# Where a fused attention and two-layer FFN kernel does its second softmax and its first split

## Chip, cores and metric

The kernel runs on one core of one Trainium2 chip. The metric is the device time of one execution in microseconds (us), from start to end. Engines are called TensorE (PE), VectorE (DVE), ScalarE (ACT), GpSimd (POOL) and SyncE (SP).

## What is computed

A window attention with given weights (a softmax over 7 taps for each token and head, then a weighted sum of 7 neighbouring tokens), and two feed-forward layers on its result:

```python
w = weight_gen - np.max(weight_gen, axis=-1, keepdims=True)
w = np.exp(w)
w = w / (np.sum(w, axis=-1, keepdims=True) + 1e-09)
x_pad = np.concatenate([np.zeros((B, pad, D)), x], axis=1)   # pad = 6
...
out = np.einsum('bshk,bskhg->bshg', w, x_unf)                # B 2, S 4096, H 8, K 7, D 192
h = x @ w_in ; g = h * np.cos(h)      ; x = g @ w_out        # first layer, 192 -> 2048 -> 192
h = x @ w_in2; g = np.maximum(0.01*h, h); out = g @ w_out2   # second layer
```

## The kernel before

The 8192 tokens lie 64 to a partition; a chunk is 4 of these (J = 4), so there are C = 16 chunks of 512 tokens. Each FFN layer works through 8 units of 256 hidden columns. Float32 products are made of high and low parts: ScalarE rounds a copy to the high part, VectorE or GpSimd subtracts it from the value for the low part, and TensorE multiplies the parts in turn. TensorE fills a slot of PSUM (`fill_alone`, or `both_products`, which interleaves the fill of one unit with the sum of the unit three before it); ScalarE and VectorE turn the slot into `gate`, then `g_hi` and `g_lo`, and `both_products` or `sum_alone` adds it into `acc_a` and `acc_b`. Each engine has its own instruction list, written out by hand; order on an engine is the order of the code, and between engines semaphores decide.

What matters here is the start, before the steady loop. SyncE issues the loads in one list: the softmax weights of chunk 0 (`load_gen(0)`), the tokens of chunk 0 (`load_own(0)`), their halo, the 6 tokens before each partition's own (`load_halo`, four transfers), the columns of the first input matrix in three pieces (`load_columns`, `HI_PIECES`), with `load_gen(1)`, the softmax weights of chunks 1 and 2, behind the first piece. GpSimd issues the loads of the first output matrix (L638) after the last piece of columns has landed.

VectorE makes the softmax of chunk 0, then the attention of chunk 0 (`attention(0, dve)`): products with the taps (L318) and additions (L327). Its first item, `start`, needs only the chunk's own tokens (three products); the second, `rest_of_window`, waits for the halo. The semaphore `att` counts these, and TensorE, which must be kept busy for its clock, runs three dummy matmuls for each (`raise_clock`, L1381). When `att` is 11, TensorE transposes the tokens into a slot (`transpose_input`). ScalarE meanwhile rounds the columns (`column_highs_a`, `column_turns`, `column_highs_b`: L861, L867, L868, L875 for each piece), then splits the transposed tokens (`split_high`: L749, L751, L755), makes the exponentials of softmax 1 (L855) and loads the sine table (L850). VectorE makes the low parts of the first unit's columns (L1092), the first two parts of softmax 1 ("max" L1068, "subtract" L1071), the low parts of the tokens (`split_low`, L938 and L941), and the rest of softmax 1: "sum" L1074, "guard" L1077, "invert" L1080, "multiply" L1083. Then the first gate follows: `whole` (ScalarE L785), fraction (VectorE L1009), sine (ScalarE L825, L828), product (VectorE L1038), `g_hi` (ScalarE L720, L723), `g_lo` (VectorE L910, L914), for which TensorE's first `both_products` waits at `wait_to_sum`. Unit 0 is handled in halves of 512 columns, the others whole (L791, L1017, L832, L1043, L732, L919).

GpSimd makes the low parts of the other columns (`column_lows`, L643), those of the output matrix in four pieces of two instructions (`out_lows`, L649), and between them parts of the attention of chunk 1 (its L318 and L327 rows, `of_pool`), which wait for softmax 1.

Of the kernel before, what the change touches and what calls it, by code (L numbers as in the profile page):

```python
# [39 lines left out]
INPUT_STEP = 16  # L40
# [16 lines left out]
def window_attention_two_ffn(nc, x, weight_gen, w_in1, w_out1, w_in2, w_out2, out):  # L57
# [20 lines left out]
    gen_rows = weight_gen.rearrange("b (p t) h k -> (b p) (t h) k", t=per_part)  # L78
# [46 lines left out]
    def fills(i, step):  # L125

        if i < 0:
            return 1
        return 1 + sum(exists(j, s) for j in range(i) for s in range(STEPS)) + sum(
            exists(i, s) for s in range(step + 1))  # L130
# [28 lines left out]
    with ctx:  # L159
        def sb(name, shape, dt=FP32):  # L160
            return ctx.enter_context(nc.sbuf_tensor(name, shape, dt))

        def sem(name):
            return ctx.enter_context(nc.semaphore(name))
# [26 lines left out]
        taps_w = sb("taps_w", [P, per_part * heads, taps])  # L191
# [34 lines left out]
        gen_loaded = [sem(f"gen{n}_loaded") for n in range(5)]  # L226
# [67 lines left out]
        HEAD_PARTS, TAIL_PARTS = ["max", "subtract"], ["sum", "guard", "invert", "multiply"]  # L294
# [112 lines left out]
        def b_pairs(b, cols):  # L407

            first = cols.start + P
            return b[:, first:first + cols.stop - cols.start]\  # L410
                .rearrange("p (u t c) -> p u t c", t=PAIR, c=P)[:, :, 0, :]

        def b_lows(b_lo, cols):
            return b_lo[:, cols.start // PAIR:cols.stop // PAIR]\
                .rearrange("p (u c) -> p u c", c=P)
# [10 lines left out]
        HI_PIECES = [slice(a * UNIT, b * UNIT) for a, b in ((0, 2), (2, 5), (5, 8))]  # L426
        LO_PIECES = [slice(a * UNIT, b * UNIT) for a, b in ((1, 2), (2, 5), (5, 8))]

        def first_lows(cols):
# [6 lines left out]
        HEAD_ROWS, SOFT_ROWS = [[slice(a * J * heads, b * J * heads) for a, b in chunks]  # L436
                                for chunks in (SOFT_HEADS, SOFT_CHUNKS)]
# [56 lines left out]
        def _(sp):  # L494
            def load_gen(n):

                rows = HEAD_ROWS[n]
                sp.dma_start(taps_w[:, rows, :], gen_rows[:, rows, :]).then_inc(gen_loaded[n], 16)
# [22 lines left out]
            load_halo(sp, 0, 0)  # L521
            load_halo(sp, 0, P // batch)
            load_columns(0)
            load_gen(1)
            load_columns(1)
            load_columns(2)
            load_out(W1, w_out1, slice(0, TILES // 2), out_loaded[0])
# [184 lines left out]
        def _(act):  # L712
            def halves(t):
                return t.rearrange("p (k n) -> p k n", k=2)
# [25 lines left out]
            def split_high(i, step, chunk):  # L740
                if chunk >= 2:
                    act.wait_ge(x_moved[0], 16 * (chunk - 1))
                    nc.scalar.activation(x1_a_hi[:, :], x_raw_a[:, :], ACT.Copy).then_inc(x1_hi, 1)
                    act.wait_ge(x_moved[1], 16 * (chunk - 1))
                    nc.scalar.activation(x1_b[0:DB, :], x_raw_b, ACT.Copy).then_inc(x1_hi, 1)
                else:
                    act.wait_ge(filled, fills(i, step))
                    slot = slots[step % SLOTS]
                    nc.scalar.activation(halves(x1_a_hi[:, :]), slot[:, :, 0:N // 2], ACT.Copy)\  # L749
                        .then_inc(x1_hi, 1)  # L750
                    nc.scalar.activation(halves(x1_b[0:DB, :]), slot[0:DB, :, N // 2:N], ACT.Copy)\  # L751
                        .then_inc(x1_hi, 1)
                if chunk <= 2:
                    act.wait_ge(x1_hi, chunk * 2 + 2)
                    nc.scalar.activation(x1_up[DB:P, :], x1_b[0:DB, :].bitcast(FP32), ACT.Copy)\  # L755
                        .then_inc(x1_up_ready, 1)
# [95 lines left out]
            def exponentials(n):  # L852
                rows = HEAD_ROWS[n]
                act.wait_ge(soft, soft_count(n, "subtract"))
                nc.scalar.activation(taps_w[:, rows, :], taps_w[:, rows, :], ACT.Exp)\  # L855
                    .then_inc(exp_ready, 1)
# [7 lines left out]
            def column_turns(n):  # L864
                cols = HI_PIECES[n]
                a_raw = W1.in_a_raw[:, cols]
                nc.scalar.activation(a_raw, a_raw, ACT.Copy, scale=PER_TURN).then_inc(w1_hi, 1)  # L867
                nc.scalar.activation(b_lows(W1.in_b_lo_raw, cols), b_pairs(W1.in_b_raw, cols), ACT.Copy,  # L868
                                     scale=PER_TURN).then_inc(w1_raw, 1)

# [5 lines left out]
                    .then_inc(w1_hi, 1)  # L876

            exponentials(0)
            act.wait_ge(padded, 2)
            for n in range(len(HI_PIECES)):  # L880
                column_highs_a(n)
                column_turns(n)
                column_highs_b(n)
            split_high(-1, INPUT_STEP, 0)
            exponentials(1)
            act.wait_ge(ident_ready, 2)
            load_sine()

# [14 lines left out]
        def _(dve):  # L903
# [181 lines left out]

            for part in HEAD_PARTS + TAIL_PARTS:
                softmax(0, part)
            for instruction in attention(0, dve):
                instruction()
            dve.wait_ge(w1_hi, 2)  # L1090
            for lo, raw, hi in first_lows(slice(0, UNIT)):
                nc.vector.tensor_tensor(lo, raw, hi, ALU.subtract).then_inc(w1_first_lo, 1)  # L1092
            for part in HEAD_PARTS:
                softmax(1, part)
            split_low(INPUT_STEP, 0)
            for part in TAIL_PARTS:
                softmax(1, part)

            of_chunk_1 = list(attention(1, dve))
            for step in range(STEPS):  # L1100
# [345 lines left out]
```

## Time and profile before

| | us |
|---|---|
| median of 3 runs (1150.20 to 1150.30) | 1150.26 |
| the profiled execution | 1151.76 |
| its span, first to last instruction | 1150.0 |
| TensorE busy | 1132.5 (98%) |
| VectorE busy | 934.6 (81%) |
| ScalarE busy | 724.9 (63%) |
| GpSimd busy | 87.1 (8%) |

The page of the profile gives busy time for each engine, the span in 40 slices of 28.75 us, and groups of instructions. All of the change lies in the first slice and the start of the second, so the timeline (every instruction with its start, its duration and what it waited for) is the view to use, beside the table of stretches, which gives each engine's busy time and the granted TensorE clock.

### The profile page before, as it was taken

The numbers are of one execution on the slowest core, as the hardware profiler recorded it, in microseconds if no ns is written. First come the engines' busy times: TensorE is split into PE (matmuls) and PEld (weight loads), VectorE is DVE, ScalarE is ACT, GpSimd is POOL, SyncE is SP. The second block draws the span as 40 slices with busy tenths as digits, with TensorE's granted clock in tenths as the row PEclk, the third lists the DMA queues.
The fourth block names the chain that finished last, engine by engine and source line by source line (L and its number), as shares of the span: only waits on it lengthen the run. The fifth ranks groups of instructions, "written<-read, shape, count | busy, mean of one in ns | idle before, by whom it ended". The sixth has DMA issues, their size and how long they took to land.

```text
span 1150.0 us, 22937 instructions
## 1 busy us (share of the span) xinstructions
PE 1132.5 (98%) x9766; PEld 996.1 (87%) x9766; DVE 934.6 (81%) x913; ACT 724.9 (63%) x775; POOL 87.1 (8%) x80
## 2 busy tenths in 40 slices
PE   7999999999999999999999999999999999999998
PEld 5778989988888888899998989988888898898976
DVE  7989798888979889697896978969798796978543
ACT  5666774766747666575665757566575665757544
POOL 5870000000000000000000000000000000000000
PEclk9999999999999999999999999999999999999999
DMA  9760201103011020201102011020201102010001
GB/s 257 203 129 1 63 2 32 45 1 77 1 37 41 1 76 1 54 24 31 47 1 76 1 36 42 4 74 1 47 31 30 48 1 77 1 37 7 1 15 29
DMA packets 85262, 48.41 MB, mean 42 GB/s; under 512 B 58156, under 2 KB 78762, under 8 KB 84776
## 3 DMA queue, kind: packets, MB, share of 16 engines
q1 hardware_dynamic: 80712, 41.70, 14.1%
q0 software_dynamic: 4448, 5.24, 2.5%
q8 instruction: 77, 1.26, 0.4%
q14 instruction: 25, 0.20, 0.1%
HBM read 35.12 MB, written 11.80 MB: 41 GB/s over the span
## 4 chain that ended last, share of the span: by engine, by line
PE 89%; DVE 4%; ACT 1%; issue 1%; ACTq 0%; DVEq 0%
PE slot L1200 41%; PE acc_a L1200 28%; PE acc_b L1200 18%; DVE g_lo L919 1%; DVE prods L327 0%; DVE prods L318 0%; ACT g_hi L732 0%; DVE gate L1017 0%; PE acc_b L1173 0%; ACT gate L795 0%; ACT L855 0%; PE acc_b L1174 0%; PE acc_a L1166 0%; PE acc_a L1165 0%; ACT taps_w L855 0%
## 5 line engine op out<-in xcount | busy, mean ns | idle before, releaser
L1200 PE MATMUL acc_a<-g_hi,out_hi_lo 64*128 64x512 f32 x2000 | 699.0, 390 | 0.0
L919 DVE TENSOR_TENSOR g_lo<-gate,g_hi 128x1024 fp32r<-128x1024 f32 x252 | 309.2, 1227 | 119.0 <-ACT g_hi L732 118.5
L1200 PE MATMUL acc_b<-g_hi,out_hi_lo 64*128 64x512 f32 x1000 | 389.6, 390 | 5.7 <-DVE g_lo L919 3.0
L1200 PEld LDWEIGHTS acc_a<-g_hi,out_hi_lo 64*128 64x128 f32 x2000 | 370.0, 185 | 26.6
L1200 PE MATMUL acc_a<-g_lo,out_hi_lo 64*128 64x512 f32 x1000 | 387.9, 388 | 0.0
L1200 PE MATMUL acc_b<-g_lo,out_hi_lo 64*128 64x512 f32 x1000 | 387.6, 388 | 0.0
L732 ACT ACTIVATE g_hi<-gate 128x1024 fp32r<-128x1024 f32 x252 | 267.3, 1061 | 97.4 <-PE acc_b L1200 78.0
L1200 PE MATMUL slot<-x_a_hi,in_a_lo 64*128 64x512 f32 x1024 | 301.8, 390 | 1.3 <-DVE g_lo L919 0.6
L1200 PE MATMUL slot<-x_a_lo,in_a_hi 64*128 64x512 f32 x1024 | 300.9, 388 | 0.4 <-DVE x_a_lo L938 0.4
L1200 PE MATMUL slot<-x_b,in_b_hi 64*128 64x512 f32 x1024 | 300.9, 388 | 0.2 <-DVE x_b L941 0.2
L1200 PE MATMUL slot<-x_a_hi,in_a_hi 64*128 64x512 f32 x1024 | 300.7, 388 | 0.0
L795 ACT ACTIVATE gate<-slot 128x1024 f32<-128x1024 f32 x128 | 130.8, 1022 | 125.4 <-PE slot L1200 99.0
L1200 PEld LDWEIGHTS acc_b<-g_hi,out_hi_lo 64*128 64x128 f32 x1000 | 184.9, 185 | 24.8 <-issue 8.9
L1200 PEld LDWEIGHTS acc_a<-g_lo,out_hi_lo 64*128 64x128 f32 x1000 | 185.3, 185 | 12.1
L1200 PEld LDWEIGHTS acc_b<-g_lo,out_hi_lo 64*128 64x128 f32 x1000 | 185.0, 185 | 10.4
L1017 DVE SCALAR_TENSOR_TENSOR gate<-slot,whole 128x1024 f32<-128x1024 f32 x127 | 155.1, 1221 | 46.8 <-ACT whole L791 46.1
L791 ACT ACTIVATE whole<-slot 128x1024 int32<-128x1024 f32 x127 | 130.1, 1024 | 72.7 <-PE slot L1200 72.7
L1200 PEld LDWEIGHTS slot<-x_a_hi,in_a_lo 64*128 64x128 f32 x1024 | 145.9, 185 | 17.4 <-PE slot L1200 2.9
L1200 PEld LDWEIGHTS slot<-x_a_lo,in_a_hi 64*128 64x128 f32 x1024 | 146.1, 185 | 13.2 <-DVE x_a_lo L938 0.8
L1200 PEld LDWEIGHTS slot<-x_b,in_b_hi 64*128 64x128 f32 x1024 | 146.1, 185 | 13.0 <-DVE x_b L941 1.0
L1200 PEld LDWEIGHTS slot<-x_a_hi,in_a_hi 64*128 64x128 f32 x1024 | 146.1, 185 | 12.0
L1043 DVE SCALAR_TENSOR_TENSOR gate<-slot,gate 128x1024 f32<-128x1024 f32 x124 | 151.6, 1222 | 6.0 <-ACT gate L832 4.1
(110 smaller groups left out, 1023.0 us busy)
## 6 DMA issues: line engine op xcount, KB each, us to landing
x_win<-in_x SPq DMA_DIRECT2D x14, 960.0 KB, 4.7
x_columns<-prods SPq DMA_DIRECT2D x56, 96.0 KB, 2.0
out<-turned_a SPq DMA_DIRECT2D x240, 16.0 KB, 1.5
x_raw_a<-x_columns SPq DMA_DIRECT2D x14, 256.0 KB, 2.8
out<-turned_b SPq DMA_DIRECT2D x120, 16.0 KB, 1.5
result<-x_columns SPq DMA_DIRECT2D x14, 128.0 KB, 3.0
out_raw<-in_moe_w_out SPq DMA_DIRECT2D x3, 512.0 KB, 8.6
out_hi_lo<-in_moe_w_out POOLq DMA_DIRECT2D x2, 768.0 KB, 10.7
```

The costliest lines, as they stand in the source:

```text
L732: nc.scalar.activation(g_hi[:, q % 2, :], result_of(i, q), ACT.Copy)\
L791: nc.scalar.activation(whole[:, q % 2, :], slot, ACT.Identity, bias=0.25)\
L795: nc.scalar.activation(gate[:, q % 2, :], slot, ACT.Prelu, alpha=0.01)\
L919: nc.vector.tensor_tensor(g_lo[:, q % 2, :], result_of(i - b, q), g_hi[:, q % 2, :].bitcast(FP32), ALU.subtract)\
L1017: nc.vector.scalar_tensor_tensor(gate[:, q % 2, :], slot, 0.25, whole[:, q % 2, :], ALU.add, ALU.subtract)\
L1043: nc.vector.scalar_tensor_tensor(result_of(i, q), slot, RADIANS, gate[:, q % 2, :], ALU.mult, ALU.mult)\
L1200: return nc.tensor.matmul(to, w[rows, :], x[rows, :], start=start, stop=stop)
```

## The change

Four things are moved; nothing is left out and no instruction is new but for the place of one.

1. The load of the softmax weights of chunks 1 and 2 leaves SyncE's list, where it stood behind the first piece of columns, and is issued by ScalarE behind its first exponentials.
2. On VectorE "max" and "subtract" of softmax 1 move ahead of the first product that waits for the halo. The exponentials of softmax 1 move on ScalarE ahead of the work on the columns.
3. On ScalarE `split_high` for the tokens of chunk 0 moves ahead of the last two instructions of the last piece of columns.
4. On VectorE "sum", "guard" and "invert" of softmax 1 stand ahead of `split_low`; "multiply" alone stays behind it.

```diff
@@ sync
             load_columns(0)
-            load_gen(1)
             load_columns(1)
@@ scalar, column_turns
                 nc.scalar.activation(a_raw, a_raw, ACT.Copy, scale=PER_TURN).then_inc(w1_hi, 1)
+                if n == len(HI_PIECES) - 1:
+                    split_high(-1, INPUT_STEP, 0)
                 nc.scalar.activation(b_lows(W1.in_b_lo_raw, cols), b_pairs(W1.in_b_raw, cols), ACT.Copy,
                                      scale=PER_TURN).then_inc(w1_raw, 1)
@@ scalar, its list
             exponentials(0)
+
+            act.dma_start(taps_w[:, HEAD_ROWS[1], :], gen_rows[:, HEAD_ROWS[1], :])\
+                .then_inc(gen_loaded[1], 16)
+            exponentials(1)
             act.wait_ge(padded, 2)
             for n in range(len(HI_PIECES)):
                 column_highs_a(n)
                 column_turns(n)
                 column_highs_b(n)
-            split_high(-1, INPUT_STEP, 0)
-            exponentials(1)
             act.wait_ge(ident_ready, 2)
             load_sine()
@@ vector
-            for instruction in attention(0, dve):
+            first, *others = attention(0, dve)
+            first()
+            for part in HEAD_PARTS:
+                softmax(1, part)
+            for instruction in others:
                 instruction()
             dve.wait_ge(w1_hi, 2)
             for lo, raw, hi in first_lows(slice(0, UNIT)):
                 nc.vector.tensor_tensor(lo, raw, hi, ALU.subtract).then_inc(w1_first_lo, 1)
-            for part in HEAD_PARTS:
+            for part in TAIL_PARTS[:-1]:
                 softmax(1, part)
             split_low(INPUT_STEP, 0)
-            for part in TAIL_PARTS:
-                softmax(1, part)
+            softmax(1, TAIL_PARTS[-1])
```

On VectorE, around the products that wait for the halo (`halo0_loaded`), the order before was:

```order
L318 TENSOR_TENSOR prods<-x_win,taps_w 128x768 [waits own0_loaded,soft]
L318 TENSOR_TENSOR prods<-x_win,taps_w 128x576
L318 TENSOR_TENSOR prods<-x_win,taps_w 128x384
L318 TENSOR_TENSOR prods<-x_win,taps_w 128x192 [waits halo0_loaded,x_zeroed]
L318 TENSOR_TENSOR prods<-x_win,taps_w 128x384
```

And with the change (a line number of the changed kernel is 3 higher in the softmax):

```order
L318 TENSOR_TENSOR prods<-x_win,taps_w 128x768 [waits own0_loaded,soft]
L318 TENSOR_TENSOR prods<-x_win,taps_w 128x576
L318 TENSOR_TENSOR prods<-x_win,taps_w 128x384
L1071 TENSOR_REDUCE scratch<-taps_w 128x64 [waits gen1_loaded]
L1074 TENSOR_TENSOR taps_w<-taps_w,scratch 128x448 [waits soft]
L318 TENSOR_TENSOR prods<-x_win,taps_w 128x192 [waits halo0_loaded,x_zeroed]
L318 TENSOR_TENSOR prods<-x_win,taps_w 128x384
```

Two instructions and a second wait, for `gen1_loaded`, now stand ahead of the product that waits for the halo.

On VectorE, from the low parts of the first columns to the first gate, before:

```order
L1092 TENSOR_TENSOR in_b_lo<-in_b_lo_raw,in_b_hi 128x128
L1068 TENSOR_REDUCE scratch<-taps_w 128x64 [waits gen1_loaded]
L1071 TENSOR_TENSOR taps_w<-taps_w,scratch 128x448 [waits soft]
L938 TENSOR_TENSOR x_a_lo<-slot,x_a_hi 128x512 [waits x1_hi]
L941 TENSOR_TENSOR x_b<-slot,x_b 64x512
L1074 TENSOR_REDUCE scratch<-taps_w 128x32 [waits exp_ready]
L1077 TENSOR_SCALAR scratch<-scratch 128x32 [waits soft]
L1080 RECIPROCAL scratch<-scratch 128x32 [waits soft]
L1083 TENSOR_TENSOR taps_w<-taps_w,scratch 128x224 [waits soft]
L1009 SCALAR_TENSOR_TENSOR gate<-slot,whole 128x512 [waits unit_act]
```

And now:

```order
L1099 TENSOR_TENSOR in_b_lo<-in_b_lo_raw,in_b_hi 128x128
L1077 TENSOR_REDUCE scratch<-taps_w 128x32 [waits exp_ready]
L1080 TENSOR_SCALAR scratch<-scratch 128x32 [waits soft]
L1083 RECIPROCAL scratch<-scratch 128x32 [waits soft]
L941 TENSOR_TENSOR x_a_lo<-slot,x_a_hi 128x512 [waits x1_hi]
L944 TENSOR_TENSOR x_b<-slot,x_b 64x512
L1086 TENSOR_TENSOR taps_w<-taps_w,scratch 128x224 [waits soft]
L1012 SCALAR_TENSOR_TENSOR gate<-slot,whole 128x512 [waits unit_act]
```

Three short instructions of softmax 1 left the place between the split and the first gate, and the two longer ones left this stretch.

On ScalarE, the last piece of columns and the split, before:

```order
L861 ACTIVATE in_a_hi<-in_a_raw 128x768 [waits in2_loaded]
L867 ACTIVATE in_a_raw<-in_a_raw 128x768
L868 ACTIVATE in_b_lo_raw<-in_b_raw 128x384
L875 ACTIVATE in_b_hi<-in_b_raw 128x768 [waits w1_raw]
L749 ACTIVATE x_a_hi<-slot 128x512 [waits filled]
L751 ACTIVATE x_b<-slot 64x512
L755 ACTIVATE x_up<-x_b 64x512 [waits x1_hi]
L855 ACTIVATE taps_w<-taps_w 128x448 [waits soft]
L850 ACT_TABLE_LOAD
```

And now:

```order
L860 ACTIVATE in_a_hi<-in_a_raw 128x768 [waits in2_loaded]
L866 ACTIVATE in_a_raw<-in_a_raw 128x768
L748 ACTIVATE x_a_hi<-slot 128x512 [waits filled]
L750 ACTIVATE x_b<-slot 64x512
L754 ACTIVATE x_up<-x_b 64x512 [waits x1_hi]
L869 ACTIVATE in_b_lo_raw<-in_b_raw 128x384
L876 ACTIVATE in_b_hi<-in_b_raw 128x768 [waits w1_raw]
L849 ACT_TABLE_LOAD
```

The split stands two instructions earlier, those two stand behind it, and the exponentials are gone from here.

## Rows read from the trace of the kernel before

**Rows 1.** What TensorE waited for over the span: total us, times, longest.

```profile
PE acc_b L1200 <- DVE g_lo L919: 3.0, 4, 1.8
```

**Rows 2.** Stretches: bounds, length, busy us of PE, PEld, DVE, ACT, POOL; clock, DMA share, GB/s.

```profile
5.00:10.00 5.00, 4.30 (x10) 3.46 (x11) 4.07 (x8) 0.00 (x0) 2.39 (x5) 1.00 1.05 225
...
31.28:33.20 1.92, 0.01 (x2) 0.00 (x0) 1.92 (x2) 1.31 (x2) 1.92 (x2) 1.00 0.54 107
34.20:37.40 3.20, 3.20 (x19) 3.08 (x17) 3.20 (x4) 1.91 (x2) 3.20 (x4) 0.50 1.08 296
42.70:43.28 0.58, 0.00 (x0) 0.00 (x0) 0.58 (x2) 0.58 (x2) 0.58 (x1) 1.00 1.19 291
```

**Rows 3.** Timeline to 12 us: start, us, engine, line, work, count, idle time before it.

```profile
3.62 0.39 ACT L855 ACTIVATE taps_w<-taps_w 128x224 f32<-128x224 f32 x1 [1.60 <-DVE taps_w L1071]
5.52 2.50 DVE L318 TENSOR_TENSOR prods<-x_win,taps_w 128x768 f32<-128x768 f32 x3
8.88 1.70 DVE L318 TENSOR_TENSOR prods<-x_win,taps_w 128x192 f32<-128x192 f32 x3 [0.86 <-DMA x_win<-in_x]
11.07 0.63 ACT L861 ACTIVATE in_a_hi<-in_a_raw 128x512 fp32r<-128x512 f32 x1 [7.06 <-DMA in_b_raw<-in_moe_w_in]
```

**Rows 4.** Transfers issued in the first 12 us: count, KB each, us to landing.

```profile
x_win<-in_x SPq DMA_DIRECT2D x2, 216.0 KB, 4.3
taps_w<-in_weight_gen SPq DMA_DIRECT2D x1, 224.0 KB, 6.3
taps_w<-in_weight_gen SPq DMA_DIRECT2D x1, 112.0 KB, 2.0
```

**Rows 5.** Timeline from 18.7 to 26.5 us, the split and softmax 1.

```profile
18.75 0.83 ACT L867 ACTIVATE in_a_raw<-in_a_raw 128x768 f32<-128x768 f32 x1
19.46 0.61 DVE L1068 TENSOR_REDUCE scratch<-taps_w 128x64 f32<-128x448 f32 x1
19.53 0.22 PE L1135 MATMUL slot<-ident,prods 64*64 64x64 f32 x2
20.11 0.62 DVE L1071 TENSOR_TENSOR taps_w<-taps_w,scratch 128x448 f32<-128x448 f32 x1
20.77 0.58 ACT L749 ACTIVATE x_a_hi<-slot 128x512 fp32r<-128x512 f32 x1
21.86 0.69 DVE L938 TENSOR_TENSOR x_a_lo<-slot,x_a_hi 128x512 fp32r<-128x512 f32 x1 [1.13 <-ACT x_b L751]
24.96 1.59 DVE L1083 TENSOR_TENSOR taps_w<-taps_w,scratch 128x224 f32<-128x224 f32 x1
25.36 1.09 ACT L785 ACTIVATE whole<-slot 128x512 int32<-128x512 f32 x2 [0.76 <-PE slot L1200]
26.47 1.27 DVE L1009 SCALAR_TENSOR_TENSOR gate<-slot,whole 128x512 f32<-128x512 f32 x2
```

**Rows 6.** Timeline from 28 us, VectorE's side and TensorE's restart.

```profile
30.50 0.71 DVE L910 TENSOR_TENSOR g_lo<-gate,g_hi 128x512 fp32r<-128x512 f32 x1
31.13 2.03 DVE L914 TENSOR_TENSOR g_lo<-gate,g_hi 128x512 fp32r<-128x512 f32 x1
33.26 0.47 PE L1200 MATMUL acc_b<-g_hi,out_hi_lo 64*128 64x512 f32 x1 [1.97 <-issue]
36.44 1.86 DVE L919 TENSOR_TENSOR g_lo<-gate,g_hi 128x1024 fp32r<-128x1024 f32 x1
```

**Rows 7.** Timeline of GpSimd from 24.4 us.

```profile
24.46 1.84 POOL L643 TENSOR_TENSOR in_a_lo<-in_a_raw,in_a_hi 128x768 fp32r<-128x768 f32 x1
28.67 1.99 POOL L649 TENSOR_TENSOR out_hi_lo<-out_raw,out_hi_lo 128x256 fp32r<-128x256 f32 x2 [1.25 <-DMA out_hi_lo<-in_moe_w_out]
29.36 1.30 POOL L649 TENSOR_TENSOR out_hi_lo<-out_raw,out_hi_lo 128x512 fp32r<-128x512 f32 x1
30.62 1.99 POOL L318 TENSOR_TENSOR prods<-x_win,taps_w 128x768 f32<-128x768 f32 x1
44.62 3.06 POOL L318 TENSOR_TENSOR prods<-x_win,taps_w 128x768 f32<-128x768 f32 x2
```

## Prediction

> **What bounds the kernel now.** TensorE is busy 98% of the span, and the view of what it waited for has few rows; the largest is 3.0 us for low parts of `g` made by VectorE, in 4 waits [rows 1]. A change at the start can therefore pay only through the moment from which TensorE runs without a gap, and whatever shift is left at 43.28 us, where TensorE restarts for the last time before the steady loop's rhythm, is carried to the end nearly one for one. So I read the table of stretches first. It shows two holes there: 31.28 to 33.2 us and 42.70 to 43.28 us, both with VectorE busy throughout [rows 2]. From 34.20 to 37.40 us the granted clock is 0.50, so 1.2 GHz instead of 2.4, after the hole of 2 us; TensorE loses 1.6 us there, but waits for VectorE again at 42.70, so that loss and its return are hidden until VectorE is earlier. The chain to shift is VectorE's, from the first gate (L1009 at 26.47) to the first `g_lo` (L910, L914), which lets TensorE restart at 33.26 [rows 5, 6].
>
> That chain has a second partner. L910 takes 0.71 us, and L914, the same work on the other half, 2.03 us, ending at 33.16 [rows 6]. GpSimd's product L318 stands at 30.62 with 1.99 us; two of them take 3.06 elsewhere, 1.53 each [rows 7]. The rows fit turns at something that the two engines share: GpSimd waits 0.45 us for L910, then L914 waits until GpSimd's instruction ends at 32.61 and takes 0.55. "Multiply" (L1083) shows the same at 24.96: 1.59 us, ending just after GpSimd's L643 that ran from 24.46 to 26.30 [rows 5, 7]. And GpSimd's own clock at this place is a landing: its L649 starts at 28.67 after 1.25 us of waiting for the first output matrix [rows 7], whose load the change doesn't move (the same bytes go ahead of it).
>
> **Part 1 and 2, weights and halo.** Call h the delay of VectorE's halo products, now at 8.88 after 0.86 us of idling [rows 3]. "Max" and "subtract" take 0.65 + 0.54 = 1.19 us up to the next instruction's start (from 19.46 to 20.11, and 0.62 less the overlap of 0.08 that VectorE's rows have) [rows 5]. VectorE is free at 8.02. If weights and halo were there, the products would start at 9.21, h = 0.33: that is the lower bound, never a gain at this point. The weights: ScalarE issues the load after its first exponentials, at 3.62 + 0.39 = 4.0 [rows 3]. From issue to landing, 112 KB took 2.0 us on the empty queue and these 224 KB took 6.3 behind the columns; halo parts of 216 KB took 4.3 in the same stretch [rows 4]. I take 4.4, nearest to the halo's, so landing at 8.4 and products at 9.6; the bounds are 8.02 or before (h = 0.33) and 10.3 (h = 2.6). The halo: the DMA engines are full here (share 1.05, 225 GB/s [rows 2]), so 224 KB put beside it cost it up to 1.0 us and, if half of them are served later, 0.5. The products would start at 9.4 to 9.9. The later of the two gives h = 0.7 to 1.0, and I take 1.0.
>
> Here the Trainium skill bears on how the halo is hit. DMA: Bandwidth & Descriptors, "Anatomy of one DMA", says that each DMA engine goes round between queues and drains a whole packet of some 9 to 17 descriptors before it switches. By that ScalarE's load would be served nearly at once and the halo bear all of it, h = 1.0 with an early landing of the weights; no row of before shows two queues side by side.
>
> All of the attention of chunk 0 is VectorE's serial work, so it ends h later. The exponentials of softmax 1 go on ScalarE at 10.1 + 0.6 = 10.7 at best, and the columns start at 11.07 [rows 3]: hidden.
>
> **Part 3, the earlier split.** TensorE's transposes end at 19.75; ScalarE splits at 20.77, because the last columns hold it [rows 5]. Now it is free at 18.75 + 0.83 = 19.58 and the split starts 0.05 after the transposes: 19.8 + h. The gain is 0.97 - h, so about 0 with h = 1.0 (from +0.64 to -1.6). VectorE's L938 goes with the split (it waited 1.13 us for it [rows 5]): the first unit's fill shifts by h - 0.97, and so does `whole` L785 at 25.36, to about 25.4. The two column instructions behind the split, 1.2 us (from 19.58 to 20.77), take the place of the exponentials, some 0.6 (0.39 for half the size [rows 3]). ScalarE had 0.76 us of idling before `whole` [rows 5], so it stays covered.
>
> **Part 4, softmax 1 out of the way.** "Sum", "guard" and "invert" now stand between 19.46 + h and L938 at 21.86: 1.4 us of room at h = 1. Before, they took at most 1.7, from the split's end (21.86 + 2 x 0.69) to 24.96, with waits in it. "Multiply" alone remains, behind the split, near 23.5, over before 24.5. VectorE's first gate no longer waits until 26.47 for it, but for the first half of `whole`, at 25.36 + 0.6 (half of 1.09 and an overlap) = 26.0, plus the shift of the fill. So the gate moves from 26.47 to 26.02 + (h - 0.97), a shift of s = h - 1.42; with h = 1.0, 0.4 us earlier. This is the gain that the change makes for sure in its own place.
>
> **What is late next.** L910 would ask at 30.50 - 0.4 = 30.1. GpSimd's L649 holds from 29.36 to 30.66 [rows 7]. By the turns above L910 runs when that ends, 30.66 to 31.2, GpSimd's L318 is next, and L914 again ends near 33.2. TensorE restarts at 33.26 as before. For every s between -1.1 (L910 ahead of the L649 of 29.36) and +0.12 (L910 still asks before GpSimd's L318 at 30.62) the shift is swallowed by that turn; that is h from 0.3 to 1.54. Sum: 0.4 us earlier at the gate, 0.4 lost at L910, 0.0 to 0.1 left. The profiled execution is 1151.76 with a span of 1150.0, 1.5 over the median of 1150.26; since the sum is 0, I set it against the median: **1150.3 us**.
>
> The Trainium skill, SBUF — State Buffer, "SBUF: two separate sides", states this as a rule: VectorE and GpSimd share a port pair, held for a whole instruction where VectorE has two SBUF inputs and GpSimd reads SBUF, and the other blocks. By this rule the 0.4 us are lost, without it L914 would come after a GpSimd product begun at 30.62 that ends at 32.15, and 0.4 us would be kept (1149.9). The trace agrees with the rule: 0.71 against 2.03 us for the same work.
>
> **Rivals.** *Late, the turn is lost* (slower side). If h is over 1.54, L910 asks after GpSimd's L318 has begun. It then runs after it, from 30.66 + 1.53 = 32.2 to 32.8, the second L318 holds to 34.3, and L914 ends at 34.9: TensorE restarts 1.7 us later. Following the next turns (L649s of 1.99 for two, L919, which took 1.86 instead of 1.21 [rows 6]) I find 2.0 us left at 43.28: 1152.3, and some way over it if the half clock lasts beyond that. It decides at a landing of the weights at 9.2, 0.8 later than I took, or a halo at 10.4. For it: queues are full and the old landing took 6.3 us; against: the load no longer stands behind the columns. 15%.
>
> *Early, past GpSimd.* If L649 doesn't hold L910 (only the L318 form does) and h is under 0.8, L914 asks before 30.62, both halves go ahead of GpSimd, TensorE restarts at 31.3, and after the next turns 1.7 us stay: 1148.6. Against it: L919 at 36.44 was held by an L649. 8%.
>
> *Kept in full.* The turns don't bind at all: s = -0.4 passes, 1149.9. 12%, and the same verdict as the forecast.
>
> *The clock falls in the front.* The dummy matmuls run dry longer, since their triggers come h later, and the first fill runs at 1.2 GHz: the 1.6 us of 34.20 to 37.40 again, before the chain, which then also loses the turn: some 3 us, 1153.3. Against: before, it took a hole of 1.92 us [rows 2] ahead of the fall. 5%.
>
> *It doesn't do what it says*: ScalarE becomes the last before `whole` and the gate stays at 26.47. Same time, 1150.3, inside the forecast.
>
> **How the numbers follow.** Forecast 60% (1149.9 to 1150.8 its own range), kept in full 12%, late 15%, early 8%, clock 5%. 0.2%, about what a measurement of this kernel can tell from no change, is 2.3 us: 1147.96 and 1152.56. Faster by more needs the early case and another half us: 5%. Slower by more: the clock case and a third of the late one, 10%. The rest, 85%, is within. The range takes in early and late at their prices: 1148.5 to 1152.5, leaving out the clock case and the outer parts of the others, some 15%.
>
> **What would show it.** Right: "max" starts between 8.2 and 8.9 us, halo products at 9.6 to 10.1, split at 20.6 to 21.0, first gate at 26.0 to 26.2, L910 either long or at 30.6, L914 again near 2 us, TensorE's restart within 0.3 us of 33.26. Wrong: halo products after 10.4 (late), a restart before 32 or after 34, a clock of 0.5 before 30 us, or a first L649 of GpSimd that starts well off 28.67, which would carry the restart with it. The sum would also fail if the holes after 43 us [rows 1] changed, which are set by turns of the same kind.

## The result: slower, by the rival that was given 15%

| | before | changed |
|---|---|---|
| median, 13 runs each | 1150.32 us (1149.79 to 1151.78) | 1153.17 us (1151.48 to 1154.86) |
| ratio, 95% interval | | 1.0022 (1.0014 to 1.0029) |
| span of the profiled execution | 1150.0 us | 1152.2 us |

The changed kernel is 2.5 us slower by the ratio. The forecast was 1150.3 with a range up to 1152.5: wrong, and on the side of the rival *late, the turn is lost*. Measured a second time, the ratio was 1.0018 (1.0010 to 1.0027), below.

The cause stands in the first 12 us. From the transfers of the changed kernel issued there (count, KB each, us from issue to landing):

```profile
x_win<-in_x SPq DMA_DIRECT2D x2, 216.0 KB, 4.1
taps_w<-in_weight_gen ACTq DMA_DIRECT2D x1, 224.0 KB, 6.7
```

The weights on ScalarE's queue took 6.7 us, no better than the 6.3 us behind the columns in [rows 4] (5.3 to 5.6 in the five later traces of kernels that issue them there). They were issued at 3.70 and landed at 10.40. The halo was not held up (4.1 after 4.3). From the timeline of the changed kernel, VectorE at that place and what follows on ScalarE:

```profile
3.70 0.38 ACTq L881 DMA_DIRECT2D taps_w<-in_weight_gen  x1
6.70 2.18 DVE L318 TENSOR_TENSOR prods<-x_win,taps_w 128x768 f32<-128x768 f32 x3
10.43 0.62 DVE L1071 TENSOR_REDUCE scratch<-taps_w 128x64 f32<-128x448 f32 x1 [1.55 <-DMA taps_w<-in_weight_gen]
11.62 1.69 DVE L318 TENSOR_TENSOR prods<-x_win,taps_w 128x192 f32<-128x192 f32 x3
22.52 0.60 ACT L748 ACTIVATE x_a_hi<-slot 128x512 fp32r<-128x512 f32 x1 [3.38 <-PE slot L1141]
25.70 1.28 ACT L849 ACT_TABLE_LOAD   x1
27.12 1.09 ACT L784 ACTIVATE whole<-slot 128x512 int32<-128x512 f32 x2
27.76 1.29 DVE L1012 SCALAR_TENSOR_TENSOR gate<-slot,whole 128x512 f32<-128x512 f32 x2 [2.21 <-ACT whole L784]
```

"Max" waits 1.55 us for the weights (VectorE was free at 8.88), and the halo products start at 11.62 instead of 8.88 [rows 3]: h = 2.74. The wait of 0.86 us for the halo is gone; in its place stands one for weights that land at 10.40, with 1.19 us of work behind it. ScalarE now idles 3.38 us before the split, so having the split two instructions earlier buys nothing here.

The records of the transfers' packets say where the 6.7 us went. ScalarE's queue is q10. Its first packet starts at 5.67, 2.0 us after the issue; most of its 144 run from 7.0 to 8.5 us, side by side with those of SyncE's queue q1 (packets, MB, share of the 16 engines in that stretch):

```profile
q1 hardware_dynamic: 131, 0.24, 58.9%
q10 hardware_dynamic: 120, 0.19, 44.9%
```

The last one ends at 9.2, and the landing is told at 10.40. So the weights weren't the last in a list, but their packets began late, shared the engines, and were reported late.

The place where TensorE restarts, from the same timeline (GpSimd, VectorE, TensorE):

```profile
22.36 0.72 POOL L642 TENSOR_TENSOR in_a_lo<-in_a_raw,in_a_hi 128x256 fp32r<-128x256 f32 x1 [2.25 <-DVE in_b_lo L1099]
28.19 1.00 POOL L642 TENSOR_TENSOR in_b_lo<-in_b_lo_raw,in_b_hi 128x384 fp32r<-128x384 f32 x1
29.16 1.99 POOL L648 TENSOR_TENSOR out_hi_lo<-out_raw,out_hi_lo 128x256 fp32r<-128x256 f32 x2
31.10 3.49 POOL L318 TENSOR_TENSOR prods<-x_win,taps_w 128x768 f32<-128x768 f32 x2
31.80 1.39 DVE L913 TENSOR_TENSOR g_lo<-gate,g_hi 128x512 fp32r<-128x512 f32 x1
33.12 2.03 DVE L917 TENSOR_TENSOR g_lo<-gate,g_hi 128x512 fp32r<-128x512 f32 x1
35.24 0.46 PE L1206 MATMUL acc_b<-g_hi,out_hi_lo 64*128 64x512 f32 x1 [2.20 <-issue]
43.78 1.21 DVE L922 TENSOR_TENSOR g_lo<-slot,g_hi 128x1024 fp32r<-128x1024 f32 x1
```

L913 asks at 31.80, after GpSimd's product has begun at 31.10, and is held too: 1.39 us where [rows 6] have 0.71. L917 then waits for GpSimd's second product. The restart comes at 35.24 instead of 33.26, 1.98 us later, although the gate before it moved by 1.29 only (27.76 against 26.47).

GpSimd itself is late too. Its low parts of the output matrix (L648) start at 29.16 where they started at 28.67, and no longer behind a landing: they follow its low parts of the columns, which could start only at 22.36, when VectorE's L1099 was done. So of the 1.98 us GpSimd's own delay is 0.49, and the lost turn is the other 1.49.

At the fourth `g_lo` (43.78; in the kernel before 42.02) 1.76 us are left.

From there the shift is carried as it is: by comparing the starts of VectorE's 257 `g_lo` instructions in the two traces, it is 1.6 to 1.8 us for the next 36. The other 0.5 us of this pair of traces came in once, near 205 us. TensorE waited there for tokens that had been late from memory, in the chain of waits of the changed kernel from 195 to 240 us (start, us, what):

```profile
194.66 4.11 DMA x_columns<-prods
198.78 3.12 DMA x_raw_a<-x_columns
```

The same transfers take 2.0 and 2.8 us as medians over the span of the kernel before, and the second trace of the changed kernel has no such wait: against the second trace of the kernel before its shift is 3.24 us at the fourth `g_lo` and still 3.26 past that place. So this 0.5 us isn't the change's.

### The profile page after: what moved, and what is told of

It is laid out like the page before. It is cut to its first block, busy times and chain, and to the rows that moved or that the text cites. A ratio compares the mean times of both kernels' runs of the same rounds, so it can differ in the third digit from the quotient of the medians.

```text
span 1152.2 us, 22937 instructions
## 1 busy us (share of the span) xinstructions
PE 1133.0 (98%) x9766; PEld 940.1 (82%) x9766; DVE 935.1 (81%) x913; ACT 725.5 (63%) x775; POOL 85.1 (7%) x80
## 4 chain that ended last, share of the span: by engine, by line
PE 87%; DVE 5%; ACT 2%; issue 1%; DMA 1%; SPq 0%; ACTq 0%; DVEq 0%
PE slot L1206 41%; PE acc_a L1206 27%; PE acc_b L1206 18%; DVE g_lo L922 2%; DVE prods L327 1%; DVE prods L318 1%; ACT g_hi L731 1%; DVE gate L1020 0%; ACT gate L794 0%; DMA x_columns<-prods 0%; PE acc_b L1179 0%; DMA x_raw_a<-x_columns 0%; DVE prods L975 0%; ACT L854 0%; PE acc_b L1180 0%
## 5 line engine op out<-in xcount | busy, mean ns | idle before, releaser
L1206 PE MATMUL slot<-x_a_hi,in_a_lo 64*128 64x512 f32 x1024 | 297.8, 389 | 0.8 <-DVE g_lo L922 0.4
L1206 PE MATMUL slot<-x_b,in_b_hi 64*128 64x512 f32 x1024 | 297.3, 388 | 0.5 <-DVE x_b L937 0.3
L1206 PE MATMUL slot<-x_a_lo,in_a_hi 64*128 64x512 f32 x1024 | 296.9, 387 | 0.0
L1206 PE MATMUL slot<-x_a_hi,in_a_hi 64*128 64x512 f32 x1024 | 296.8, 387 | 0.0
L1206 PEld LDWEIGHTS slot<-x_a_hi,in_a_lo 64*128 64x128 f32 x1024 | 142.2, 184 | 22.6 <-PE slot L1206 2.9
L1206 PEld LDWEIGHTS slot<-x_b,in_b_hi 64*128 64x128 f32 x1024 | 142.3, 185 | 20.0 <-DVE x_b L944 1.0
L1206 PEld LDWEIGHTS slot<-x_a_lo,in_a_hi 64*128 64x128 f32 x1024 | 142.3, 184 | 18.5 <-DVE x_a_lo L941 0.2
L1206 PEld LDWEIGHTS slot<-x_a_hi,in_a_hi 64*128 64x128 f32 x1024 | 142.3, 184 | 17.9
```

Source lines behind the costliest of these rows:

```text
L1206: return nc.tensor.matmul(to, w[rows, :], x[rows, :], start=start, stop=stop)
```

## The experiments

Each kernel is compared with the kernel before on the same chip; a ratio is to that, with its 95% interval.

### Both kernels again, without an edit

> The changed kernel, unchanged, for a second trace of it. Theory: the weights land at 9.4 to 10.8 (three traces with this queue gave 9.4 to 10.8), the restart stands 6.1 us behind the start of GpSimd's first low parts of the output matrix (the turn is lost), and is 2 to 3.5 us later than in the second trace of the kernel before; ratio 1.002. Rival (the first trace was an unlucky one): the landing is near 8.4 here and the restart 4.6 us behind.

> The kernel before, unchanged, for a second trace of it. Turn theory: TensorE's restart stands 4.6 us behind the start of GpSimd's first low parts of the output matrix where L910 is asked before GpSimd's L318 begins, and 6.1 to 6.3 behind it where it is asked later; in the first trace it was 4.59. So the restart is 4.6 or 6.1 to 6.3 behind it here, by which of the two comes first, and not anything between. Rival (restart follows the first gate): restart 6.8 us behind the first gate, as in the first trace, whatever GpSimd does. Ratio 1.000.

Measured: the changed kernel 1.0018 (1.0010 to 1.0027), the kernel before against itself 1.0004 (0.9995 to 1.0013). In the second trace of the changed kernel the weights again take 6.7 us, "max" starts at 10.61, the first low part is asked at 31.98 and the restart comes at 35.45. So the first trace was typical.

The first trace of the kernel before was not, in one point at least. In its second trace, VectorE's "guard" of softmax 0 and the products, then ScalarE and VectorE at the split:

```profile
4.57 1.15 DVE L1077 TENSOR_SCALAR scratch<-scratch 128x32 f32<-128x32 f32 x1
6.70 3.79 DVE L318 TENSOR_TENSOR prods<-x_win,taps_w 128x768 f32<-128x768 f32 x6
19.69 0.60 ACT L749 ACTIVATE x_a_hi<-slot 128x512 fp32r<-128x512 f32 x1 [0.42 <-PE slot L1135]
23.31 0.76 DVE L1083 TENSOR_TENSOR taps_w<-taps_w,scratch 128x224 f32<-128x224 f32 x1
24.93 1.29 DVE L1009 SCALAR_TENSOR_TENSOR gate<-slot,whole 128x512 f32<-128x512 f32 x2 [0.86 <-ACT whole L785]
```

The six products run through without a wait: the idle time of 0.86 us, into which the change puts "max" and "subtract", isn't there. The halo's last part had landed at 8.04, and not at 8.79 as in the first trace. Of six traces of kernels with the loads of the kernel before, five have it between 7.8 and 8.1, and the wait in them is 0.07 us at most.

ScalarE waits 0.42 us for the transposes: the columns had landed earlier, and it was done with them. "Multiply" takes 0.76 us, not 1.59, and VectorE idles 0.86 us before the first gate. The 0.97 us that I gave part 3 and the 0.45 us that I gave part 4 were there to win in the first trace [rows 5] and not in this one. Neither is the rule: in the trace of the hold with the moved product, near the end of the experiments, whose VectorE has the order of the kernel before up to here, the split comes late again and "multiply" is long:

```profile
20.77 0.69 DVE L939 TENSOR_TENSOR x_a_lo<-slot,x_a_hi 128x512 fp32r<-128x512 f32 x1 [0.98 <-ACT x_b L752]
24.00 1.60 DVE L1084 TENSOR_TENSOR taps_w<-taps_w,scratch 128x224 f32<-128x224 f32 x1
```

In the second trace of before the first gate is at 24.93, and against that the changed kernel's (27.94 in its second trace) is 3.0 us late. The restart is at 32.00, so the changed kernel's is 3.45 us late: GpSimd's low parts came 1.96 us later (29.36 and 27.40), and the lost turn cost 1.49 again. The spans differ by 3.4 us (1147.4 and 1150.8), those of the first pair by 2.3; over many runs the two ratios make it 2.5 and 2.1.

### What the restart hangs on

The turns, taken together with the first traces, say that the restart follows GpSimd's low parts with one of two distances. All traces without a hold on GpSimd, from the rows of GpSimd's first low parts (L649, L648 in the changed kernel), its first product (L318), VectorE's first low part, and TensorE's restart, in us:

| kernel | GpSimd's low parts | GpSimd's product | low part asked | restart | restart less low parts |
|---|---|---|---|---|---|
| before, first trace | 28.67 | 30.62 | 30.50 | 33.26 | 4.59 |
| before, second trace | 27.40 | 29.36 | 28.97 | 32.00 | 4.60 |
| weights first | 27.64 | 29.85 | 29.31 | 32.25 | 4.61 |
| behind the halo | 28.14 | 30.07 | 30.33 | 34.22 | 6.08 |
| ScalarE early | 27.91 | 29.84 | 30.55 | 34.01 | 6.10 |
| split only | 27.90 | 30.03 | 30.81 | 34.17 | 6.27 |
| softmax only | 28.11 | 30.07 | 31.23 | 34.21 | 6.10 |
| one copy more | 28.04 | 29.99 | 31.19 | 34.14 | 6.10 |
| changed, first trace | 29.16 | 31.10 | 31.80 | 35.24 | 6.08 |
| changed, second trace | 29.36 | 31.31 | 31.98 | 35.45 | 6.09 |

Ten traces, two distances, and the sign of "asked less product" tells which without a miss. (In "split only" the product itself waited 0.16 us for its tokens.) That sign decides the 1.5 us; when GpSimd's low parts start, from 27.40 to 29.36 here, moves the restart one for one. The rival that the restart stands 6.8 us behind the first gate fails: 32.00 less 24.93 is 7.07, and 35.24 less 27.76 is 7.48. "Behind the halo" is the closest one: asked 0.26 us too late, it pays 1.5.

The delay by itself, on the kernel before:

```diff
             for part in HEAD_PARTS:
                 softmax(1, part)
+            dve.wait_ge(x1_hi, 2)
+            nc.vector.tensor_copy(turned_a[:, :].rearrange("p (k n) -> p k n", k=2),
+                                  slots[INPUT_STEP % SLOTS][:, :, 0:N // 2])
             split_low(INPUT_STEP, 0)
```

> The kernel before with one more copy on VectorE (128x512 from PSUM, 0.7 us) ahead of the low parts of the tokens, whose result nobody reads. All of the chain to the first low part comes 0.7 us later. Turn theory: the restart doesn't move by 0.7 but by 0 or 1.5, so it stands 4.6 or 6.1 us behind the start of GpSimd's first low parts of the output matrix; with the second trace of before (L910 asked 0.39 ahead of GpSimd's product) the turn is lost: 6.1, restart near 33.5. Rival (shifts carry as they are): restart 32.7, 5.3 behind.

Measured: restart 34.14, 6.10 behind, as the turns say, and not 32.7. But it isn't a clean test of 0.7 us, since the low part was asked at 31.19, 2.2 us later than in the second trace of before: "multiply" fell into another GpSimd instruction (1.58 us) and `whole` of the second unit came late (1.10 us of idling before L1017). Ratio 1.0006 (0.9997 to 1.0015), unclear.

Taking GpSimd away, on the kernel before:

```diff
+            pool.wait_ge(lo_ready, 1)
             for instruction in of_pool[:2]:
                 instruction()
             out_lows(1)
```

> The kernel before with one wait added on GpSimd: its two products of chunk 1 start only when the first unit's low parts are done, so that L914 has no GpSimd instruction against it. Turn theory: L914 takes 0.7 instead of 2.03 us, TensorE restarts at 31.8 to 31.9 instead of 33.26; the turns that follow come later, and 0.9 to 1.2 us of it are left at 43 us: 1149.2, ratio 0.999. Rival (L914 is long for another reason): restart at 33.26, L914 still near 2 us. Rival (gain given back when GpSimd's later work comes late): restart early, but ratio 1.000.

Timeline, VectorE, GpSimd and TensorE with the hold:

```profile
28.98 1.10 DVE L911 TENSOR_TENSOR g_lo<-gate,g_hi 128x512 fp32r<-128x512 f32 x1
30.00 0.68 DVE L915 TENSOR_TENSOR g_lo<-gate,g_hi 128x512 fp32r<-128x512 f32 x1
30.76 3.77 POOL L318 TENSOR_TENSOR prods<-x_win,taps_w 128x768 f32<-128x768 f32 x2 [1.23 <-DVE g_lo L915]
30.78 0.47 PE L1201 MATMUL acc_b<-g_hi,out_hi_lo 64*128 64x512 f32 x1 [0.57 <-issue]
46.79 3.53 POOL L327 TENSOR_TENSOR prods<-prods 128x1536 f32<-128x1536 f32 x1
48.89 2.24 DVE L318 TENSOR_TENSOR result<-x_win,taps_w 128x768 f32<-128x768 f32 x1
```

The second half takes 0.68 us instead of 2.03, and the restart is 1.2 us earlier than in the second trace of before (30.78, 32.00). L911, which has only GpSimd's low parts against it, is still held (1.10), so these hold it too: that speaks against the rival *early, past GpSimd*. I had expected 31.8 to 31.9 against the first trace, where GpSimd's low parts came 1.1 us later. But the ratio is 0.9999 (0.9990 to 1.0008). The last rows say why: VectorE's product at 48.89 now falls into GpSimd's L327, which ends at 50.32, and takes 2.24 us instead of 0.95. What one turn gave, a later one took.

The same hold on the changed kernel:

> The changed kernel with GpSimd's two products of chunk 1 held until the first unit's low parts are done. Turn theory: L913 is not or hardly blocked, L917 takes 0.7 instead of 2.03 us, TensorE restarts 1.9 us earlier against the first gate (5.5 to 5.9 us behind it instead of 7.5); of it about 1 is left at 43 us: ratio 1.0005 to 1.0015 instead of 1.0022. Rival (the turn matters little): 1.002.

Measured: both halves take 0.68 and 0.69 us, the restart is at 33.52, 5.44 us behind the first gate instead of 7.48; ratio 1.0012 (1.0003 to 1.0021). The same later product takes 2.25 us. The point estimate moved as the turns say; the intervals overlap.

### Which part costs

The weights issued by SyncE ahead of the halo, all else as changed:

```diff
             load_own(0)
+            load_gen(1)
             load_halo(sp, 0, 0)
...
-            act.dma_start(taps_w[:, HEAD_ROWS[1], :], gen_rows[:, HEAD_ROWS[1], :])\
-                .then_inc(gen_loaded[1], 16)
             exponentials(1)
```

> The changed kernel, with the softmax weights of chunks 1 and 2 issued by SyncE behind the chunk's own tokens and ahead of the halo, instead of by ScalarE. Theory (the whole loss is the landing of these weights at 10.40 us, and what VectorE's shift does after it): weights land near 6.2, the halo up to 1.0 later than before, so at 9.8 at most; halo products start at 9.2 to 9.9 instead of 11.62; the shift of the first low part is under 0 and is swallowed by GpSimd's turn; TensorE restarts at 33.2 to 33.4, ratio to the kernel before 1.000. Rival (the new order on VectorE costs by itself, wherever the weights come from): restart near 35, ratio 1.002. Rival (no turns, shifts carry as they are): restart 32.8, ratio 0.9996.

Its timeline and its row of transfers:

```profile
7.96 0.61 DVE L1070 TENSOR_REDUCE scratch<-taps_w 128x64 f32<-128x448 f32 x1
9.14 1.69 DVE L318 TENSOR_TENSOR prods<-x_win,taps_w 128x192 f32<-128x192 f32 x3
```

```profile
taps_w<-in_weight_gen SPq DMA_DIRECT2D x1, 224.0 KB, 4.0
```

The landing takes 4.0 us from an earlier issue, "max" starts when VectorE is free, and the products 0.34 us later than in the second trace of before. Neither weights nor halo is waited for. The restart, which I had expected at 33.2 to 33.4, came at 32.25, since GpSimd's low parts started at 27.64. Ratio 1.0006 (0.9997 to 1.0014): of 2.5 us some 1.8 are gone.

The 0.34 us flatter the order, though. "Guard" of softmax 0 took 0.24 us in this trace and 1.15 in the second trace of before. In the other kernel with its weights first (the last one below) it took 1.14, and the products start at 9.97, 1.17 us later than in that trace of before (8.80):

```profile
8.79 0.61 DVE L1071 TENSOR_REDUCE scratch<-taps_w 128x64 f32<-128x448 f32 x1
9.97 1.69 DVE L318 TENSOR_TENSOR prods<-x_win,taps_w 128x192 f32<-128x192 f32 x3
```

So where "guard" is held, the two instructions cost their full 1.19 us even with the weights there, since there is no wait for the halo left to fill. That is h = 1.2 without any late landing, and by the turns that kernel would lose the next one if it had no hold on GpSimd: its low part is asked at 30.14, and GpSimd's low parts are done at 29.50, when its product could start. How often that happens in the runs behind the 1.0006 isn't known.

The queue kept, the moment moved, by issuing ahead of the first exponentials:

```diff
+            act.dma_start(taps_w[:, HEAD_ROWS[1], :], gen_rows[:, HEAD_ROWS[1], :])\
+                .then_inc(gen_loaded[1], 16)
             exponentials(0)
-
-            act.dma_start(taps_w[:, HEAD_ROWS[1], :], gen_rows[:, HEAD_ROWS[1], :])\
-                .then_inc(gen_loaded[1], 16)
             exponentials(1)
```

> The changed kernel, with the weights still on ScalarE's queue but issued before the first exponentials, near 0.7 us instead of 3.7. Theory (the moment counts, not the queue): they land near 6, halo products start at 9.1 to 9.9 instead of 11.62, ratio 1.000 to 1.001. Rival (a second queue on the same DMA engines is served late, 6.7 us from its issue whatever is ahead): landing near 7.5, products at 9.1 too, but the first softmax's own weights not delayed. Rival (it takes bandwidth from the first weights and the chunk's tokens): first max at 3.5 or later instead of 2.8.

```profile
taps_w<-in_weight_gen ACTq DMA_DIRECT2D x1, 224.0 KB, 3.3
taps_w<-in_weight_gen SPq DMA_DIRECT2D x1, 112.0 KB, 3.5
```

Issued on empty queues, the same transfer on the same queue takes 3.3 us, not 6.7. So the queue as such isn't slow; the moment is. The third theory held as well: the first weights take 3.5 us instead of 2.0, the first "max" starts at 4.25 instead of 2.8, and the halo products at 10.38 because of that, over the 9.1 to 9.9 that I had expected. Ratio 1.0010 (1.0002 to 1.0019).

"Max" and "subtract" behind the halo products, the load as changed:

```diff
             first()
+            for instruction in others[:2]:
+                instruction()
             for part in HEAD_PARTS:
                 softmax(1, part)
-            for instruction in others:
+            for instruction in others[2:]:
                 instruction()
```

> The changed kernel, with max and subtract two items later on VectorE, behind the products that wait for the halo; the weights are on ScalarE's queue as in the changed kernel. Theory: the halo products start at 8.9 again, the wait for the weights (landing 9.4 to 10.4) is covered by them, and of the delay of 2.7 us only the two instructions' own 1.2 are left: split 1.0 to 1.5 us earlier than in the changed kernel, ratio to the kernel before 1.000 to 1.001. Rival (moving the two instructions ahead costs the same wherever they stand): 1.002.

Measured: "max" at 9.71 without a wait, split at 21.06, 1.46 us earlier than in the changed kernel, as expected. But the low part was asked 0.26 us too late and the turn was lost: 1.0015 (1.0006 to 1.0024), over what I had expected, by the one step that I had left out there.

The softmax part alone, and the split alone (each diff is that part of the change):

> The kernel before with the softmax part alone: weights on ScalarE's queue, max and subtract ahead of the halo products, exponentials ahead of the columns; the split and the rest of softmax 1 where they were. Theory (the loss is the late landing): weights land near 10.4, halo products at 11.6, restart of TensorE near 35.2, 2 to 3 us over the kernel before, ratio 1.0022, the same as the whole change. Rival (the earlier split, with ScalarE's two column instructions behind it, makes `whole` late in the changed kernel): this kernel is about 1 us faster than the changed one.

> The kernel before with the earlier split alone: ScalarE splits the tokens ahead of the last two instructions of the columns, the exponentials stay behind them. Turn theory: the split starts at 19.8 instead of 20.77, the first gate near 25.5 instead of 26.47 (softmax 1 or ScalarE's table then last), L910 asks at 29.6 but waits for GpSimd until 30.66, L914 still ends near 33.2: restart 33.26 within 0.2, ratio 1.000. Rival (shifts carry): restart near 32.3, ratio 0.9992.

Softmax alone: 1.0019 (1.0010 to 1.0028). The weights take 5.8 us here, the products start at 10.60, the restart is 6.10 behind. That is the whole loss, within the intervals; the rival (the split costs 1 us more) isn't supported, and with intervals 2 us wide it isn't excluded. The landing, expected near 10.4, was at 9.38.

Split alone: 1.0013 (1.0004 to 1.0022), where I expected 1.000. It starts at 19.70, where it also starts in the second trace of before. What it changes is what follows. Timeline of ScalarE, VectorE and GpSimd:

```profile
22.77 0.56 ACT L855 ACTIVATE taps_w<-taps_w 128x448 f32<-128x448 f32 x1
23.36 0.39 DVE L1075 TENSOR_REDUCE scratch<-taps_w 128x32 f32<-128x224 f32 x1 [1.15 <-ACT taps_w L855]
23.79 1.85 POOL L643 TENSOR_TENSOR in_a_lo<-in_a_raw,in_a_hi 128x768 fp32r<-128x768 f32 x1
23.78 1.90 DVE L1078 TENSOR_SCALAR scratch<-scratch 128x32 f32<-128x32 f32 x1
26.78 1.27 DVE L1010 SCALAR_TENSOR_TENSOR gate<-slot,whole 128x512 f32<-128x512 f32 x2
```

The two column instructions put the exponentials 1.3 us later, VectorE waits 1.15 us, "guard" lands on a GpSimd instruction and takes 1.90 instead of 0.23, and the gate is 1.85 us later than in the second trace of before. So part 3 needs part 4 and 2 to be free. The two halves lose 0.0019 and 0.0013, together more than the whole change, which fits that each by itself loses the same turn (restarts at 34.21 and 34.17, 6.1 and 6.3 behind GpSimd's low parts).

### A version with the turns out of the way

The hold, and VectorE's product that had been caught at 48.89 moved to the next step:

```diff
                 if (i, step) == (0, ATT_END + 1):
-                    for instruction in of_chunk_1[ATT_POOL + 1:]:
+                    for instruction in of_chunk_1[ATT_POOL:]:
...
-                if step == ATT_END:
-                    of_chunk_1[ATT_POOL]()
```

> The kernel before with GpSimd's two products held until the first unit's low parts are done, and VectorE's product for the last tap of chunk 1 moved from the end of step 5 to step 6, behind the fraction: where the hold was tried alone, that product took 2.24 instead of 0.95 us, against GpSimd's L327, and the gain of the earlier restart was gone. Theory: the product takes 0.95, the low part of unit 6 starts 1.0 to 1.4 us earlier against the restart than with the hold alone, ratio 0.9988 to 0.9993. Rival (another wait takes it, `whole` of step 6 is not there yet, so the move buys nothing): ratio 1.000.

> The changed kernel with the weights issued by SyncE ahead of the halo, and with the hold and the moved product of the run before. Theory: without the late landing and without turns against L910 and L914, what is left of the change is halo products 0.3 us later against 1.0 us less work between attention and first gate; first gate within 0.4 us of the kernel before's, ratio 0.9988 to 0.9995, not better than the hold and the moved product alone by more than 0.0003. Rival (the change's own idea pays once the turns are out of the way): 0.998 to 0.9987.

Measured: 0.9992 (0.9983 to 1.0001) on the kernel before, 0.9992 (0.9984 to 1.0000) on the changed one with its weights first. The product takes 0.95 us in both; the first kernel's `g_lo` of unit 6 stands 22.84 us behind the restart, after 23.32 with the hold alone: under half of what I expected, since `whole` isn't there for 0.72 us, as the rival said. The two are alike, so the change's own idea adds nothing that shows. (The changed one has its first gate at 26.09, 1.16 us later than the second trace of before and 0.38 earlier than the first.) Some 0.9 us of gain is likely but not shown; neither interval is clear of 1.

## Why the prediction was wrong, step by step

- **The failing step is the landing of the weights.** "I take 4.4, nearest to the halo's": it measured 6.7, 6.7, 5.8, 5.9 and 7.0 in the five traces with that issue. With the landing at 10.40 (I had 8.4, and 10.3 as the outer bound) h was 2.74 where I took 1.0. The row at 6.3 us in [rows 4] was the same bytes in the same traffic, 1.5 us later, and I argued it away because they no longer stood behind the columns in a list. The DMA engines were full (share 1.05 [rows 2]). The halo's cost of "0.5 to 1.0" was wrong the other way: its last part landed at 7.7 to 7.9 in four of the five traces and at 8.8 in one, no later than the 7.8 to 8.8 of the kernels with the old loads.
- The rule on queues that I put beside it stands in the Trainium skill, DMA: Bandwidth & Descriptors, "Queues, rings and completion order" (and not in the section that I named): each DMA engine goes round between queues and drains a whole packet of one before it turns to the next. The trace fits it from 7.0 to 8.5 us, where both queues have packets. What I made of it, served nearly at once and at the halo's cost, failed: the first packet came 2.0 to 2.8 us after the issue in the five traces, most of them well after that, and the landing was told 0.7 to 1.2 us after the last. Why the packets came so late isn't known.
- **On VectorE and ScalarE everything behind h held.** With h = 2.74 the prediction's formulas give the split at 19.8 + h = 22.54 (measured 22.52), `whole` at 25.36 + h - 0.97 = 27.13 (27.12), the gate at 26.02 + h - 0.97 = 27.79 (27.76), and the low part asked 1.32 later (1.30). ScalarE was just covered, with nothing to spare.
- **GpSimd's start did not hold.** I had it fixed by a landing "whose load the change doesn't move". At h = 2.74 VectorE's L1099 releases GpSimd so late that its own work ends behind that landing: 0.49 us of the first pair of traces, 1.96 of the second.
- **The turns held** in ten traces. The threshold at h = 1.54 is that of one trace, and no run tests its size. The Trainium skill, SBUF — State Buffer, "SBUF: two separate sides", states the mechanism, and the trace agrees: 0.68 us without GpSimd's product against it, 2.03 with it.
- **The rival's price was near, its chance wrong.** I priced the restart 1.7 us later and 2.0 us left at 43 us; measured 1.98 and 1.76. Some of that is luck: the turn alone cost 1.49, and the rest was GpSimd's delay, which I hadn't priced. Its end, 1152.3, is 0.9 us under the median. It had 15%. The range ended 0.7 us short of the median.
- **A second error hid behind the first**: the sum used one trace, in which halo and columns had landed late. In the other trace of before the wait for the halo and the gains of parts 3 and 4 don't exist. With h = 1.0 as I took it, the gate against that trace would have been 1.1 us late (26.05 and 24.93). The low part would have been asked near 30.1, after GpSimd's product at 29.36, and the turn lost even with the weights landing as I took it. That part of the forecast, "swallowed by that turn", was right for one trace only.

## What to carry to other kernels

A wait is no free slot: an instruction put into it brings its own wait. If its data come over the same full DMA engines at nearly the same moment, the time that they took to land before is a better estimate than a neighbour's: here 5.3 to 6.3 us before, 5.8 to 7.0 after, and 4.4 in my sum. And the wait itself may be that of one trace, as it was here. Where two engines take turns at something, a small shift is either swallowed or paid several times over, so ask which side of the next turn it ends on, and in more than one trace. Before paying for a gain, look for the next place where the same two engines meet.

## What the runs showed of the hardware that I had not expected

- A load issued second on another queue, when the DMA engines are full, took 5.8 to 7.0 us for 224 KB in five traces and cost the halo ahead of it nothing that shows; issued at once on idle engines it took 3.3 us and delayed a load issued beside it from 2.0 to 3.5.
- A VectorE instruction of 32 elements (0.2 us alone) took 1.90 us against a GpSimd instruction of 1.85. The first softmax's "guard" meets GpSimd's fill of `g_hi`, which runs from 4.59 to 5.55. In the five traces where "guard" started between 4.43 and 4.51 it took 0.18 to 0.24 us; in the eight where it started between 4.53 and 4.73 it took 0.98 to 1.18 and ended at 5.7. So 0.1 us in the landing of the first weights moves VectorE by 0.9. In the changed kernel (4.53) that was hidden by the wait for the second weights.
- The granted clock doesn't follow the hole in the same way each time. From the stretches of 28 to 45 us, the kernel before in its first and in its second trace (columns as in [rows 2]):

```profile
28.00:45.00 17.00, 14.34 (x106) 12.19 (x104) 16.78 (x15) 10.88 (x13) 15.36 (x10) 0.90 1.02 242
```

```profile
28.00:45.00 17.00, 13.30 (x110) 10.68 (x112) 17.00 (x14) 10.50 (x12) 16.03 (x11) 1.00 1.00 258
```

In both, a hole of 1.8 to 2.0 us stands before the restart; the clock fell to 1.2 GHz for a while in the first and stayed at 2.4 GHz in the second. The two traces of the changed kernel differ in the same way (0.90 and 1.00). It goes with a part of the spread of 2 to 4 us between runs of one kernel: the 59 runs on record whose mean granted clock was 0.998 or less were 1.05 us longer, in the mean, than the other runs of the same kernel on the same chip. The others, at 0.999 or 1.000, still spread by up to 4 us.
